# Attention of an fp32 kernel: three products of rounded halves over 128 rows, or whole fp32 over two groups of 64 rows

## The chip, the cores and the metric

One core of a Trainium2 chip runs the whole program in one launch. The metric is the device time of that core in microseconds (us), median of three executions.

## The reference

Attention with rotary embedding, then a mixer of four matrix products. Shapes: 4 batches, 8 heads, 576 positions, head size 64, all float32; the mixer has a hidden size of 256 over positions and of 1536 over channels.

```python
q_rot, k_rot = rotate(q), rotate(k)
scores = (1 / sqrt(64)) * q_rot @ k_rot^T
attn = exp(scores - max(scores));  attn = attn / (sum(attn) + 1e-9)
x = attn @ v                                   # to (4, 576, 512)
u = x + (relu(x^T @ w_tok1) @ w_tok2)^T
out = u + relu(u @ w_ch1) @ w_ch2
```

## The kernel before

The program has two stages, written out by hand with semaphores: attention (function `attention`) and the mixer (function `mixer`, which the change leaves as it is except for the point at which the last sums of attention are taken). Attention runs over 16 pairs `p` of heads, A and B. The 576 queries of each head are 4.5 tiles of 128, so a pair has nine tiles `i`: 0 to 3 are A's, 5 to 8 are B's, and tile 4 holds the last 64 queries of both. Each engine has its own list of steps for a pair, and the order in those lists is the schedule; nothing else moves work.

The steps of a pair are these.

- GpSimd (POOL) rotates q and k (`rotate`, L354 to L362), splits v into halves (`split_v`), and divides the result by the sums (`normalise`).
- TensorE (PE) turns q and k (`transposes`, L585, five matmuls of 128 rows and 128 columns each). ScalarE (ACT) copies what was turned, rounded to fp32r (`t_part_hi`), and VectorE (DVE) takes the rest (`t_part_lo`). Five DMAs per head then lay out `key` (rounded half of k over its rest, 128 rows) and `q_hi`, `q_cross`.
- PE makes the scores of a tile (`score`, L624): four fp32r matmuls of 288 columns, six for tile 4. DVE takes the maximum (`maximum`, L997), ACT the exponent with its sum (`exponent`, L847).
- PE turns the probabilities of the tile (`turn`, L634, four 128 by 128 transposes in fp32; `turn_tails`, L644, for the last 64 keys of two or three tiles at once). ACT copies them rounded (`turned_hi`, L854, and `tails_hi`), DVE takes the rest (`turned_lo`, L1005, and `tails_lo`).
- PE multiplies with v (`values`, L657): v with its rounded half and its rest side by side is the stationary operand, the turned probabilities stream past in four parts of 256 or 320 columns, nine fp32r matmuls each. ACT copies the result (`copy_o`), PE turns it back (`transpose_o`, L383), DVE adds the two halves (`sum_o`).

The score tiles use two PSUM slots of two banks (`slot`); everything else uses the four banks of `rest`, so that several turned tiles can be on their way at once, and `values` of a pair runs during the scores of the next pair. The sums of the last pair are taken inside the mixer (`last_o`, `last_sums`).

A float32 that is rounded to fp32r keeps its upper half; the two halves are multiplied as three products (upper by upper, upper by rest, rest by upper).

```python
passes = ((q_hi[a][:, cols], key[a]), (q_cross[a][:, cols], key[a]))
for n, (queries, keys) in enumerate(passes):
    for f in range(2):
        mm = pe.matmul(s[:, f, 0:HALF], queries, keys[:, f * HALF:(f + 1) * HALF], ...)
```

Of the kernel before, what the change touches and what calls it, by code (L numbers as in the profile page):

```python
# [17 lines left out]
P = 128  # L18
# [3 lines left out]
G = 4  # L22
# [39 lines left out]
def build(nc, q, k, v, w_tok1, w_tok2, w_ch1, w_ch2, rope, x_scratch, out):  # L62
    with ExitStack() as whole:
# [14 lines left out]
        with ExitStack() as placed:  # L78
            sb(placed, "w_ch1_first", [P, CT // 2, CH])
            prob_a = sb(placed, "prob_a", [P, G + 1, S])  # L80
# [61 lines left out]
Attention = namedtuple("Attention", "sync gpsimd tensor scalar vector last_o last_sums last_store buffers_left values_left slot_left")  # L142
# [85 lines left out]
def attention(nc, ctx, whole, sb, slot, rest, ident, stage_or_x, raw_qk, rope_sb, rope_half, prob_a, token, wt1, wt2, w1, x_stored,  # L228
# [7 lines left out]

# [8 lines left out]
    GROUPS = ((0, 2), (2, 5), (5, 7), (7, 9))  # L245
    PARTS = {"A0": (0, 2 * P), "A1": (2 * P, S), "B0": (S, S + HALF + TAIL // 2), "B1": (TILES * P - 2 * P, TILES * P)}
    PV_BANK = {"A0": 0, "A1": 0, "B0": 0, "B1": 2}
    O_BANKS, K_BANKS, Q_BANKS = 1, 2, 2
    EARLY = 2
    EARLY_COLS = (slice(0, EARLY * P), slice(EARLY * P, MAIN))  # L250
    LATE_COLS = slice(EARLY * P, W)

# [3 lines left out]
    rot = {"k": sb(ctx, "rot_k", [P, NG, 2, D])}  # L256
    ot = sb(ctx, "ot", [P, TILES * P])
    O_TILES = {"A": (0, G), "B": (G, TILES)}
    o_sum = {h: sb(ctx, f"o_sum_{h}", [P, O_TILES[h][1] - O_TILES[h][0], D]) for h in "AB"}

    WIDE = {"q": W, "k": S}
    t_hi = {n: [sb(ctx, f"t_hi_{n}{i}", [P, WIDE[n]], F32R) for i in range(2)] for n in "qk"}
    t_lo = {n: [sb(ctx, f"t_lo_{n}{i}", [P, WIDE[n]], F32R) for i in range(2)] for n in "qk"}
    key = [sb(ctx, f"key{a}", [P, S], F32R) for a in range(2)]
    q_cross = [sb(ctx, f"q_cross{a}", [P, MAIN], F32R) for a in range(2)]
    q_hi = [sb(ctx, f"q_hi{a}", [P, MAIN], F32R) for a in range(2)]
# [3 lines left out]
    total = [sb(ctx, f"total{a}", [P, TILES]) for a in range(2)]  # L270
    guarded = [sb(ctx, f"guarded{a}", [P, TILES]) for a in range(2)]
    inverse = [sb(ctx, f"inverse{a}", [P, TILES]) for a in range(2)]
    zeros = sb(ctx, "zeros", [P, NG, D])
    eps = sb(ctx, "eps", [P, TILES])

    rot["q"] = sb(ctx, "rot_q", [P, NG, 2, D])
    raw["v"] = sb(ctx, "raw_v", [P, 2, NG, D])
    prob_b = sb(ctx, "prob_b", [P, G, S])
    prob = [prob_a[:, i, :] for i in range(G + 1)] + [prob_b[:, i, :] for i in range(G)]
    v_sb = [sb(ctx, f"v{a}", [P, NG, P], F32R) for a in range(2)]  # L280
    pt_lo = sb(ctx, "pt_lo", [P, G, TILES * P], F32R)
    pt_hi = sb(ctx, "pt_hi", [P, NG, TILES * P], F32R)
# [4 lines left out]

    tables = sem("rope_tables")
    products = sem("products")
    rotated = sem("rotated")  # L290
    v_hi_done, v_split = sem("v_hi_done"), sem("v_split")
    consts, zero_halves = sem("consts"), sem("zero_halves")
    t_ready, t_hi_done, t_lo_done = ({n: sem(f"{what}_{n}") for n in "kq"} for what in ("t_ready", "t_hi_done", "t_lo_done"))
    tiles_in = [sem(f"tiles_in{a}") for a in range(2)]
    k1_in = sem("k1_in")
    first_turned, first_hi, first_lo = sem("first_turned"), sem("first_hi"), sem("first_lo")

    scores, maxed, exped = sem("scores"), sem("maxed"), sem("exped")
    turned, hi_done, lo_done = sem("turned"), sem("turned_hi_done"), sem("turned_lo_done")
    tails_turned, tails_hi_done, tails_lo_done = sem("tails_turned"), sem("tails_hi_done"), sem("tails_lo_done")  # L300
    pv_ready, ot_done = ({f: sem(f"{what}_{f}") for f in PARTS} for what in ("pv_ready", "ot_done"))
    o_ready, o_summed = ({h: sem(f"{what}_{h}") for h in "AB"} for what in ("o_ready", "o_summed"))
    x_done = sem("x_done")
    guard_done, inv_done = sem("guard_done"), sem("inv_done")
# [4 lines left out]
    ASSEMBLED = 5 * 16  # L309
    STORED = 3 * 16  # L310
    src = {n: a.rearrange("b (g h) s d -> (b g) h s d", h=2) for n, a in (("q", q), ("k", k), ("v", v))}

# [4 lines left out]
    def columns(bank, n):  # L317

        return rest[:].rearrange("p a n -> p (a n)")[:, bank * BANK:bank * BANK + n]

    def first_q(n0, n1):

        if n1 <= EARLY * P:
            return columns(3, n1)[:, n0:n1]
        return columns(2, n1 - EARLY * P)[:, n0 - EARLY * P:n1 - EARLY * P]

    k1_early = prob_b[:].rearrange("p a n -> p (a n)")[:, 0:W].rearrange("p (h t d) -> p h t d", h=2, t=NG)
# [8 lines left out]
    def rotate(eng, n, p):  # L336
# [20 lines left out]
        if p > 0:  # L357
            eng.wait_ge(t_ready[n], p)
        r = rot[n][:].rearrange("p t h d -> p h t d")
        eng.tensor_tensor(r[:, :, :, 0:half], by_cos[:, :, :, 0:half], by_sin[:, :, :, half:D],  # L360
                           ALU.subtract).then_inc(rotated, 1)
        eng.tensor_tensor(r[:, :, :, half:D], by_sin[:, :, :, 0:half], by_cos[:, :, :, half:D],  # L362
                           ALU.add).then_inc(rotated, 1)
# [11 lines left out]

# [3 lines left out]

    def turn_o(pe, h, bank):  # L380

        for n, t in enumerate(range(*O_TILES[h])):
            mm = pe.transpose(columns(bank, W)[:, n * P:(n + 1) * P], ot[:, t * P:(t + 1) * P], ident[:])  # L383
        mm.then_inc(o_ready[h], 1)

    def o_halves(h, bank):

        n = O_TILES[h][1] - O_TILES[h][0]
        return columns(bank, n * P).rearrange("p (t i d) -> p t d i", t=n, i=2)
# [17 lines left out]
    def sync(sp):  # L407
# [14 lines left out]
        def halves(a):  # L422
            top, low = slice(0, D), slice(D, P)
            return (top, low) if a == 0 else (low, top)

        def assemble_q(a, p):

            if no(p):
                return
            i = p % 2  # L430
            mine, other = halves(a)
            sp.wait_ge(t_hi_done["q"], p + 1)
            sp.dma_start(f32(q_hi[a][mine, :]), f32(t_hi["q"][i][mine, 0:MAIN])).then_inc(tiles_in[a], 16)
            sp.dma_start(f32(q_cross[a][other, :]), f32(t_hi["q"][i][mine, 0:MAIN])).then_inc(tiles_in[a], 16)
            sp.wait_ge(t_lo_done["q"], p + 1)
            sp.dma_start(f32(q_cross[a][mine, :]), f32(t_lo["q"][i][mine, 0:MAIN])).then_inc(tiles_in[a], 16)

        def assemble_k(a, p):

            if no(p):  # L440
                return
            i = p % 2
            mine, other = halves(a)
            sp.wait_ge(t_hi_done["k"], p + 1)
            sp.dma_start(f32(key[a][mine, :]), f32(t_hi["k"][i][mine, :])).then_inc(tiles_in[a], 16)
            sp.wait_ge(t_lo_done["k"], p + 1)
            sp.dma_start(f32(key[a][other, :]), f32(t_lo["k"][i][mine, :])).then_inc(tiles_in[a], 16)
# [18 lines left out]
        assemble_k(1, 0)  # L466
        assemble_q(1, 0)
        load("v", 0)
        load_next("k", 2)
        load_next("q", 2)  # L470

        for p in range(N):
            if p > 0:
                sp.wait_ge(v_split, 2 * p)
                load("v", p)
            store(p - 2)
            sp.wait_ge(scores, p * TILES + G)
            assemble_k(0, p + 1)
            assemble_q(0, p + 1)
            load_next("k", p + 3)  # L480
            if p > 0:
                load_next("q", p + 3)
            sp.wait_ge(scores, (p + 1) * TILES)
            assemble_k(1, p + 1)
            assemble_q(1, p + 1)
            if p == 0:
                load_next("q", p + 3)
# [14 lines left out]
        store(N - 2)  # L502

    def gpsimd(pool):
        pool.memset(ident[:], 0.0).then_inc(consts, 1)
        pool.memset(zeros[:], 0.0).then_inc(consts, 1)
        pool.memset(eps[:], 1e-9).then_inc(consts, 1)
        pool.wait_ge(consts, 3)
# [3 lines left out]
        def split_v(p, h):  # L512

            if no(p):
                return
            a = "AB".index(h)
            pool.wait_ge(raw_in["v"], (p + 1) * RAW["v"])
            if p > 0:
                pool.wait_ge(pv_ready[h + "0"], p)
                pool.wait_ge(pv_ready[h + "1"], p)  # L520
            pool.tensor_tensor(v_sb[a][:, :, 0:D], raw["v"][:, a], zeros[:], ALU.add).then_inc(v_hi_done, 1)
            pool.wait_ge(v_hi_done, 2 * p + a + 1)
            pool.tensor_tensor(v_sb[a][:, :, D:P], raw["v"][:, a], f32(v_sb[a][:, :, 0:D]),
                               ALU.subtract).then_inc(v_split, 1)

        def guard(p):

            if no(p):
                return
            pool.wait_ge(exped, (p + 1) * TILES)  # L530
            if p >= 2:
                pool.wait_ge(inv_done, p - 1)
            pool.tensor_tensor(guarded[p % 2][:], total[p % 2][:], eps[:], ALU.add).then_inc(guard_done, 1)

        def normalise(p, h):

            if no(p):
                return
            a = "AB".index(h)
            pool.wait_ge(inv_done, p + 1)  # L540
            pool.wait_ge(o_summed[h], p + 1)
            if h == "B" and p > 0:
                pool.wait_ge(x_stored, p * STORED)
            t0, t1 = O_TILES[h]
            pool.tensor_tensor(x_pair[:, 1 - a:NG, a, :], o_sum[h][:],
# [1464 lines left out]
```

## Time and profile before

| | |
|---|---|
| median of 3 executions (range) | 639.42 us (639.29 to 639.71) |
| the profiled execution: its own time, its span | 639.26 us, 637.4 us |
| PE busy, share of the span, instructions | 621.5 us, 98%, 4724 |
| PE weight loads busy | 604.5 us, 95%, 4724 |
| DVE busy | 509.9 us, 80% |
| ACT busy | 465.2 us, 73% |
| POOL busy | 341.4 us, 54% |
| DMA: bytes, mean rate | 62.32 MB, 98 GB/s |

Busy time counts the stretch in which an instruction is recorded on its engine. Matmuls overlap, and each is recorded with its latency, so what a matmul costs is read from the distance between two starts, not from its own duration. The same holds to a smaller degree for the other engines. The profiled execution lies 1.9 us outside its span and 0.2 us under the median.

### The profile page before, as it was taken

To read this page: it belongs to the slowest core of one execution; us is meant where nothing else is said; L and a number is where in the kernel's file an instruction comes from. 1 tells how busy PE (TensorE), PEld (TensorE's weight loads), DVE (VectorE), ACT (ScalarE), POOL (GpSimd) and SP (SyncE) were. 2 spreads that over 40 slices of the span, in tenths; PEclk is the share of its full clock that TensorE was granted. 3 is DMA by queue.
4 is the path that set the end of the run, shared out by engine and by line. 5 is a ranking of instruction groups with operands and counts; after the bars stand their busy time and mean duration, and the time that the engine had idled before them with its cause. 6 is when DMAs were issued, how large, how long until landed. Compare 5 with 4: busy or idle time off the path is not lost.

```text
span 637.4 us, 13799 instructions
## 1 busy us (share of the span) xinstructions
PE 621.5 (98%) x4724; PEld 604.5 (95%) x4724; DVE 509.9 (80%) x881; ACT 465.2 (73%) x1018; POOL 341.4 (54%) x316
## 2 busy tenths in 40 slices
PE   4899999999999999999999999999999999999997
PEld 3799999999999999999999999999999999999997
DVE  7899999999999999977385985569935499553895
ACT  5888999988888999976383655776556765567753
POOL 4999999998888887551900002860017800068200
PEclk9999999999999999999999999999999999999999
DMA  4667766676668765406002331000320003100002
GB/s 130 177 152 205 199 161 169 170 188 172 168 180 212 206 172 127 110 20 217 20 1 64 136 99 60 1 2 2 84 75 0 0 0 82 48 27 2 0 3 74
DMA packets 59594, 62.32 MB, mean 98 GB/s; under 512 B 16592, under 2 KB 43856, under 8 KB 59536
## 3 DMA queue, kind: packets, MB, share of 16 engines
q1 hardware_dynamic: 59232, 61.50, 35.4%
q8 instruction: 34, 0.56, 0.3%
q14 instruction: 24, 0.20, 0.1%
q10 hardware_dynamic: 304, 0.07, 0.0%
HBM read 30.77 MB, written 9.44 MB: 63 GB/s over the span
## 4 chain that ended last, share of the span: by engine, by line
PE 95%; DVE 1%; POOL 1%; ACT 1%; issue 0%
PE slot L624 12%; PE rest L657 12%; PE rest L634 9%; PE slot L1359 8%; PE slot L1361 8%; PE slot L1360 8%; PE rest L1359 6%; PE rest L1361 6%; PE rest L1360 6%; PE rest L383 3%; PE rest L585 3%; PE rest L644 2%; PE slot L1391 2%; PE rest L1391 2%; PE rest L224 1%; PE rest L221 1%
## 5 line engine op out<-in xcount | busy, mean ns | idle before, releaser
L1350 POOL TENSOR_TENSOR w_ch_part<-w_ch_sums,w_ch_part 128x512 fp32r<-128x512 f32 x21 | 31.0, 1476 | 173.3 <-ACT w_ch_part L1603 173.3
L997 DVE TENSOR_REDUCE neg_max<-slot 128x1 f32<-128x576 f32 x142 | 106.7, 752 | 6.3 <-PE slot L624 2.0
L1667 ACT ACTIVATE pieces<-h 128x288 fp32r<-128x288 f32 x168 | 73.8, 444 | 49.8 <-PE slot L1361 24.5
L1005 DVE TENSOR_TENSOR pt_lo<-rest,pt_hi 128x512 fp32r<-128x512 f32 x144 | 96.0, 677 | 1.8 <-ACT pt_hi L854 1.3
L657 PE MATMUL rest<-pt_hi,v 128*128 128x256 f32 (+1 forms) x320 | 89.3, 303 | 0.0
L854 ACT ACTIVATE pt_hi<-rest 128x512 fp32r<-128x512 f32 x144 | 84.1, 596 | 5.1 <-PE rest L634 4.2
L1758 DVE TENSOR_TENSOR pieces<-h,pieces 128x288 fp32r<-128x288 f32 x168 | 74.4, 453 | 9.3 <-ACT pieces L1667 8.8
L657 PE MATMUL rest<-pt_lo,v 128*128 128x256 f32 (+1 forms) x256 | 69.7, 295 | 0.0
L847 ACT ACTIVATE prob_a<-slot,neg_max 128x576 f32<-128x576 f32 x78 | 57.9, 743 | 9.8 <-DVE neg_max L997 9.6
L624 PE MATMUL slot<-key,q_hi 128*128 128x288 f32 x252 | 63.5, 333 | 1.5 <-ACT prob_a L847 0.5
L657 PEld LDWEIGHTS rest<-pt_hi,v 128*128 128x128 f32 x320 | 60.3, 188 | 0.2
L624 PE MATMUL slot<-key,q_cross 128*128 128x288 f32 x252 | 54.0, 296 | 0.0
L657 PEld LDWEIGHTS rest<-pt_lo,v 128*128 128x128 f32 x256 | 48.3, 189 | 0.0
L847 ACT ACTIVATE prob_b<-slot,neg_max 128x576 f32<-128x576 f32 x64 | 47.4, 741 | 0.3 <-DVE neg_max L997 0.2
L354 POOL TENSOR_TENSOR by_cos<-raw_qk,rope_sb 128x640 f32<-128x640 f32 x29 | 45.3, 1561 | 2.0
L634 PE MATMUL rest<-ident,prob_a 128*128 128x128 f32 x320 | 45.5, 273 | 0.6 <-DVE t_lo_q L986 0.5
L1825 DVE TENSOR_TENSOR h<-h 128x288 f32<-128x288 f32 x96 | 42.6, 452 | 3.9 <-ACT h L1566 3.8
L355 POOL TENSOR_TENSOR by_sin<-raw_qk,rope_sb 128x640 f32<-128x640 f32 x29 | 45.5, 1569 | 0.0
L624 PEld LDWEIGHTS slot<-key,q_hi 128*128 128x128 f32 x252 | 38.6, 193 | 3.1 <-ACT prob_a L847 1.0
L624 PEld LDWEIGHTS slot<-key,q_cross 128*128 128x128 f32 x252 | 40.5, 190 | 0.0
L634 PEld LDWEIGHTS rest<-ident,prob_a 128*128 128x128 f32 x320 | 37.9, 141 | 1.4 <-DVE t_lo_q L986 0.7
L634 PE MATMUL rest<-ident,prob_b 128*128 128x128 f32 x256 | 38.3, 273 | 0.4 <-DVE pt_lo L1005 0.2
(268 smaller groups left out, 2109.3 us busy)
## 6 DMA issues: line engine op xcount, KB each, us to landing
key<-t_hi_k SPq DMA_DIRECT2D x31, 144.0 KB, 2.3
key<-t_lo_k SPq DMA_DIRECT2D x31, 144.0 KB, 2.4
raw_qk<-in_q_dram SPq DMA_DIRECT2D x16, 256.0 KB, 2.6
raw_v<-in_v_dram SPq DMA_DIRECT2D x16, 256.0 KB, 3.1
x_scratch<-x_pair SPq DMA_DIRECT2D x16, 256.0 KB, 2.2
stage_or_x<-x_scratch SPq DMA_DIRECT2D x16, 256.0 KB, 4.1
q_hi<-t_hi_q SPq DMA_DIRECT2D x31, 128.0 KB, 2.4
q_cross<-t_hi_q SPq DMA_DIRECT2D x31, 128.0 KB, 2.4
```

The source lines that it names most:

```text
L624: mm = pe.matmul(s[:, f, 0:HALF], queries, keys[:, f * HALF:(f + 1) * HALF], start=(n == 0), stop=(n == len(passes) - 1))
L634: mm = pe.transpose(rest[:, bank, j * P:(j + 1) * P], prob[i][:, j * P:(j + 1) * P], ident[:])
L657: mm = pe.matmul(rest[:, PV_BANK[f], 0:n1 - n0], v_sb[a][:, j, :], pt[:, j, n0:n1], start=(j == 0 and pt is pt_hi), stop=(j == NG - 1))
L847: act.activation(prob[i].rearrange("p (f n) -> p f n", f=2), s[:, :, 0:HALF], ACT.Exp, bias=neg_max[p % 2][:, i:i + 1], accum_out=total[p ...
L854: act.activation(pt_hi[:, 0:G, i * P:(i + 1) * P], rest[:, bank, :].rearrange("p (j n) -> p j n", j=G), ACT.Copy).then_inc(hi_done, 1)
L997: dve.tensor_reduce(neg_max[p % 2][:, i:i + 1], slot[g if 2 <= g < 4 else g % 2][:, :, 0:HALF], AX.XY, ALU.max, negate=True).then_inc(maxe ...
L1005: dve.tensor_tensor(pt_lo[:, :, cols], rest[:, bank, :].rearrange("p (j n) -> p j n", j=G), f32(pt_hi[:, 0:G, cols]), ALU.subtract).then_i ...
L1359: pe.matmul(ps, lhs[0], rhs[0], start=first, stop=False, skip_group_check=True)
L1360: pe.matmul(ps, lhs[0], rhs[1], start=False, stop=False, skip_group_check=True)
L1361: return pe.matmul(ps, lhs[1], rhs[0], start=False, stop=last, skip_group_check=True)
L1667: act.activation(pieces[:, ring(m), 0, :], source[WEIGHTS[n]][:, ft, :], ACT.Copy).then_inc(piece_hi, 1)
L1758: dve.tensor_tensor(pieces[:, ring(m), 1, :], source[WEIGHTS[n]][:, ft, :], f32(pieces[:, ring(m), 0, :]), ALU.subtract).then_inc(piece_lo, 1)
```

## The change

Attention is written anew, with the same pairs and tiles. Every matmul of it, transposes too, now uses 64 rows of the array, and neighbours use the upper and the lower 64 rows in turn and write to different PSUM banks. No operand is split into halves.

- Scores: two fp32 matmuls of 288 columns per tile (four for tile 4). For half of the keys q and k are used where the transposition left them, for the other half a copy in the other 64 partitions, made by one DMA for q and one for k per head (`move`).
- Turned tiles: ten transposes of 64 rows by 128 columns with a 64 by 64 identity (`half_turn`), all into `rest[:, 0:2]`. One copy of 128 x 640 takes a tile out, on ACT for tiles 0, 2, 4, 6, 8 and on DVE for 1, 3, 5, 7 (`copy_turned`); the next tile is turned once that copy is done. q and k are turned into the two score slots, in line with the tiles.
- Values: the turned probabilities are now the stationary operand, 64 rows of 128 columns, and v streams past with a column of ones (65 columns), so that the sum of the exponents comes out beside the result and nothing is turned back. A pair has 90 such matmuls, into `rest[:, 2:4]`, one bank for each group of rows; DVE adds the two banks (`sum_o`), after head A's tiles and after head B's.
- The copies of v, q and k are single, the halving by ACT and DVE and the reads of the accumulated sums are gone, `last_o` and `last_sums` too.

```diff
-                    mm = pe.matmul(s[:, f, 0:HALF], queries, keys[:, f * HALF:(f + 1) * HALF],
-                                   start=(n == 0), stop=(n == len(passes) - 1))
+                for r, (x, w) in enumerate((own(0), other(1)) if a == 0 else (other(0), own(1))):
+                    mm = pe.matmul(s[:, r, 0:HALF], x[:, cols], w, start=True, stop=True, skip_group_check=True)
...
+        def half_turn(to, x, r):
+            rows = (top, low)[r]
+            return pe.matmul(to, x, ident[rows, rows], start=True, stop=True, is_transpose=True, skip_group_check=True)
...
-        def turn(p, i, bank):
+        def turn(p, i):
...
+                copied(pe, g - 1)
+            pe.wait_ge(exped, g + 1)
...
-            for j in range(G):
-                mm = pe.transpose(rest[:, bank, j * P:(j + 1) * P], prob[i][:, j * P:(j + 1) * P], ident[:])
+            for j in range(NG):
+                for r, rows in enumerate((top, low)):
+                    at = j * P if j < G or (i in UPPER and (i, r) != (G, 0)) else S - P
+                    x = wide[i][rows, at:at + P]
+                    mm = half_turn(rest[:, r, j * D:(j + 1) * D], x, r)
...
-                for pt in ((pt_hi, pt_lo) if j < G else (pt_hi,)):
-                    mm = pe.matmul(rest[:, PV_BANK[f], 0:n1 - n0], v_sb[a][:, j, :], pt[:, j, n0:n1],
-                                   start=(j == 0 and pt is pt_hi), stop=(j == NG - 1))
+            elif i == 0:
+                pe.wait_ge(o_summed["B"], p)
...
+                return pe.matmul(rest[:, 2 + r, at:at + V], x[rows, j, :], w[rows, j, :], start=begins, stop=ends, skip_group_check=True)
...
+        for p in range(N):
+            score(p, 0)
+            turn(p - 1, 7)
+            values(p - 1, 6)
             score(p, 1)
+            turn(p - 1, 8)
+            values(p - 1, 7)
             score(p, 2)
+            turn(p, 0)
+            values(p - 1, 8)
+            transposes("k", p + 1)
+            turn(p, 1)
+            values(p, 0)
             score(p, 3)
+            turn(p, 2)
             score(p, 4)
+            values(p, 1)
+            turn(p, 3)
             score(p, 5)
+            values(p, 2)
+            transposes("q", p + 1)
+            turn(p, 4)
+            values(p, 3)
             score(p, 6)
+            score(p, 7)
+            turn(p, 5)
+            values(p, 4)
             score(p, 8)
+            turn(p, 6)
+            values(p, 5)
...
-            dve.tensor_tensor(pt_lo[:, :, cols], rest[:, bank, :].rearrange("p (j n) -> p j n", j=G),
-                              f32(pt_hi[:, 0:G, cols]), ALU.subtract).then_inc(lo_done, 1)
+            dve.tensor_copy(pt_of(p, i)[:].rearrange("p j (r n) -> p j r n", r=2),
+                            banks_by_rows(rest[:, 0:2])).then_inc(by_dve_done, 1)
```

On PE, here is one stretch of a pair before, from the third score tile to the first part of the values (rows of `rest` from `pt_hi`, `pt_lo` are the products with v).

```order
L624 MATMUL slot<-key,q_hi 128x288 [waits exped]
L624 MATMUL slot<-key,q_hi 128x288
L624 MATMUL slot<-key,q_cross 128x288 x2
L657 MATMUL rest<-pt_hi,v 128x256 [waits turned_lo_done,tails_lo_done,v_split]
L657 MATMUL rest<-pt_lo,v 128x256
L657 MATMUL rest<-pt_hi,v 128x256
```

The same place now: from the third score tile of a pair to its first values.

```order
L611 MATMUL slot<-turned_k,turned_q 128x288 [waits exped]
L611 MATMUL slot<-moved_k,moved_q 128x288
L550 MATMUL rest<-ident,prob_a 128x64 [waits exped,turned_copied_by_act]
L550 MATMUL rest<-ident,prob_a 128x64 x9
L653 MATMUL rest<-v,pt 128x65 [waits turned_copied_by_act]
L653 MATMUL rest<-v,pt 128x65 x9
L550 MATMUL slot<-ident,rot_k 128x64 [waits rotated,exped]
L550 MATMUL slot<-ident,rot_k 128x64 x9
L550 MATMUL rest<-ident,prob_a 128x64 [waits exped,turned_copied_by_act]
L550 MATMUL rest<-ident,prob_a 128x64 x9
L653 MATMUL rest<-v,pt 128x65 [waits v_copied,o_summed_B,turned_copied_by_act]
L653 MATMUL rest<-v,pt 128x65 x7
```

Each turned tile now waits for the copy of the one before it, and the values of tile 0 wait for the sum of the pair before.

On DVE before, the steps of a pair after the second and third maximum (L997), down to the sixth.

```order
L997 TENSOR_REDUCE neg_max<-slot 128x1 [waits scores] x2
L1013 TENSOR_TENSOR pt_hi<-rest,pt_hi 64x384 [waits tails_hi_done]
L989 TENSOR_TENSOR t_lo_k<-rest,t_hi_k 128x576 [waits t_hi_done_k]
L1005 TENSOR_TENSOR pt_lo<-rest,pt_hi 128x4x128 [waits turned_hi_done]
L997 TENSOR_REDUCE neg_max<-slot 128x1 [waits scores]
L1005 TENSOR_TENSOR pt_lo<-rest,pt_hi 128x4x128 [waits turned_hi_done]
L986 SCALAR_TENSOR_TENSOR t_lo_q<-rest,t_hi_q 128x640 [waits t_hi_done_q]
L997 TENSOR_REDUCE neg_max<-slot 128x1 [waits scores]
```

And now, from the maxima of tiles 1 and 2 to that of tile 5.

```order
L844 TENSOR_REDUCE neg_max<-slot 128x1 [waits scores] x2
L864 TENSOR_REDUCE y_B<-rest 128x325 [waits x_done,o_added]
L836 COPY turned_k<-slot 128x640 [waits tiles_in1,tiles_in0,t_ready_k]
L854 COPY pt<-rest 128x640 [waits o_added,turned]
L872 TENSOR_TENSOR guarded<-y_B,eps 128x5 [waits o_summed_B]
L844 TENSOR_REDUCE neg_max<-slot 128x1 [waits scores]
L881 RECIPROCAL inverse<-guarded 128x5 [waits x_done,guard_done]
L844 TENSOR_REDUCE neg_max<-slot 128x1 [waits scores]
L854 COPY pt<-rest 128x640 [waits o_added,turned]
L844 TENSOR_REDUCE neg_max<-slot 128x1 [waits scores]
```

The sum of head B, the copy of k and the copy of turned tile 1 now stand in one row on DVE, between the maxima of tiles 2 and 3.

## Rows read from the trace of the kernel before

**Rows 1.** The page's first part: busy time, share of the span, instructions

```profile
PE 621.5 (98%) x4724; PEld 604.5 (95%) x4724; DVE 509.9 (80%) x881; ACT 465.2 (73%) x1018; POOL 341.4 (54%) x316
```

**Rows 2.** Windows: one pair, attention, mixer; busy us (x instructions), clock, DMA share, GB/s

```profile
150.43:167.59 17.16, 17.16 (x140) 16.65 (x139) 16.58 (x27) 15.27 (x38) 14.54 (x16) 1.00 0.70 181
12.00:297.00 285.00, 281.95 (x2215) 270.20 (x2214) 267.99 (x434) 255.61 (x611) 234.57 (x238) 1.00 0.63 166
297.00:637.40 340.40, 336.14 (x2501) 331.68 (x2499) 233.13 (x427) 204.44 (x401) 103.55 (x69) 1.00 0.13 40
```

**Rows 3.** Chain that ended last, over one pair: shares, then pieces (start us, us, what)

```profile
by line: PE slot L624 31.2%; PE rest L657 27.7%; PE rest L634 22.9%; PE rest L383 6.7%; PE rest L585 6.4%; PE rest L644 5.7%; issue 0.0%
...
150.43 0.55 PE rest L585 x5
150.97 0.44 PE rest L634 x4
...
153.43 0.52 PE slot L624 x4
...
160.97 1.07 PE rest L657 x9
```

**Rows 4.** Groups of weight loads by shape: count, busy us, mean ns of one

```profile
L624 PEld LDWEIGHTS slot<-key,q_hi 128*128 128x128 f32 x252 | 38.6, 193 | 3.1 <-ACT prob_a L847 1.0 <-DMA q_cross<-t_lo_q 0.9 <-issue 0.7
L634 PEld LDWEIGHTS rest<-ident,prob_b 128*128 128x128 f32 x256 | 29.8, 141 | 1.4 <-DVE pt_lo L1005 0.5 <-ACT ot L874 0.4
L644 PEld LDWEIGHTS rest<-ident,prob_b 128*64 128x64 f32 x64 | 6.9, 110 | 0.8
```

**Rows 5.** Timeline: two loads behind each other after a wait, transposes, then fp32r

```profile
287.83 0.20 PEld L634 LDWEIGHTS rest<-ident,prob_b 128*128 128x128 f32 x2 [0.41 <-ACT ot L874]
...
17.60 0.30 PEld L624 LDWEIGHTS slot<-key,q_hi 128*128 128x128 f32 x2 [0.42 <-ACT prob_a L847]
```

**Rows 6.** Timeline: two matmuls of a score tile, and the maximum that waits for them

```profile
17.98 0.43 PE L624 MATMUL slot<-key,q_cross 128*128 128x288 f32 x2
...
18.44 0.76 DVE L997 TENSOR_REDUCE neg_max<-slot 128x1 f32<-128x576 f32 x1 [0.78 <-PE slot L624]
```

**Rows 7.** Timeline of DVE: steps without a wait between them

```profile
153.12 0.75 DVE L997 TENSOR_REDUCE neg_max<-slot 128x1 f32<-128x576 f32 x1
153.78 0.68 DVE L1005 TENSOR_TENSOR pt_lo<-rest,pt_hi 128x512 fp32r<-128x512 f32 x1
154.38 0.81 DVE L986 SCALAR_TENSOR_TENSOR t_lo_q<-rest,t_hi_q 128x640 fp32r<-128x640 f32 x1
155.11 0.75 DVE L997 TENSOR_REDUCE neg_max<-slot 128x1 f32<-128x576 f32 x1
```

**Rows 8.** Timeline of ACT: steps without a wait between them

```profile
153.47 0.71 ACT L834 ACTIVATE t_hi_q<-rest 128x640 fp32r<-128x640 f32 x1
154.07 0.74 ACT L847 ACTIVATE prob_a<-slot,neg_max 128x576 f32<-128x576 f32 x1
154.69 0.20 ACT L847 ACTIVATION_READ_ACCUMULATOR prob_a<-slot,neg_max 128x1 f32 x1
```

**Rows 9.** Groups of DVE and POOL by shape: count, busy us, mean ns of one

```profile
L1022 DVE TENSOR_REDUCE o_sum_B<-rest 128x320 f32<-128x640 f32 x15 | 12.4, 825 | 1.6 <-PE rest L383 1.5
L355 POOL TENSOR_TENSOR by_sin<-raw_qk,rope_sb 128x640 f32<-128x640 f32 x29 | 45.5, 1569 | 0.0
L360 POOL TENSOR_TENSOR rot_q<-by_cos,by_sin 128x320 f32<-128x320 f32 x15 | 13.2, 883 | 1.2
L521 POOL TENSOR_TENSOR v<-raw_v,zeros 128x320 fp32r<-128x320 f32 x32 | 28.0, 875 | 15.6 <-PE rest L657 15.6
L545 POOL TENSOR_TENSOR x_pair<-o_sum_B,inverse 128x320 f32<-128x320 f32 x16 | 11.6, 725 | 17.4 <-DVE o_sum_B L1128 13.5 <-issue 4.0
```

**Rows 10.** Timeline of PE: the nine transposes of the last result, in the mixer

```profile
299.54 1.15 PE L383 MATMUL rest<-ident,ot 128*128 128x128 f32 x9
```

More of the change, by code:

```diff
@@ L277, in attention @@
+    rot["q"][0] = sb(ctx, "rot_q0", [P, NG, 2, D])
     raw["v"] = sb(ctx, "raw_v", [P, 2, NG, D])
[L278 to L282, printed above, removed]
+    prob_b = sb(ctx, "prob_b", [P, G * S + 2 * TAIL])
+    starts = {0: 0, 1: S, 2: 2 * S + TAIL, 3: 3 * S + TAIL, G: 4 * S + 2 * TAIL, 5: 0, 6: S, 7: 2 * S + TAIL, 8: 3 * S + TAIL}
@@ L420, in load_next, with move @@
             load(n, p)
[L422 to L426, printed above, removed]
+        def move(n, a, p):
             if no(p):
                 return
[L430 to L447, printed above, removed]
+            here, there = ((top, low), (low, top))[a]
+            sp.wait_ge(t_done[n], p + 1)
+            sp.dma_start(moved_x[n][there, :], turned_x[n][p % 2][here, MOVED_COLS[n][a]]).then_inc(tiles_in[a], 16)
         def store(p):
@@ L612, in score, with own, other @@
+            queries, keys = (turned_x[n][p % 2] for n in "qk")
+            def own(r):
+                rows = (top, low)[r]
+                return queries[rows], keys[rows, r * HALF:(r + 1) * HALF]
+            def other(r):
+                rows = (top, low)[r]
+                return moved_x["q"][rows], moved_x["k"][rows, :]
             if i == G:
-                cols, b = slice(MAIN, W), p % 2
-                passes = ((t_hi["q"][b][:, cols], t_hi["k"][b]), (t_hi["q"][b][:, cols], t_lo["k"][b]),
-                          (t_lo["q"][b][:, cols], t_hi["k"][b]))
+                cols = slice(MAIN, W)
+                for n, halves in enumerate(((own(0), other(1)), (other(0), own(1)))):
+                    for r, (x, w) in enumerate(halves):
+                        mm = pe.matmul(s[:, r, 0:HALF], x[:, cols], w, start=(n == 0), stop=(n == 1), skip_group_check=True)
@@ L635, in turn, with values @@
             mm.then_inc(turned, 1)
[L637 removed]
+        def values(p, i):
             if no(p):
                 return
[L641 to L659 removed]
@@ L728, in tensor @@
+            mm.then_inc(o_added, 1)
+        pe.wait_ge(consts, 2)
+        transposes("k", 0)
+        transposes("q", 0)
+        for p in range(N):
+            score(p, 0)
+            turn(p - 1, 7)
+            values(p - 1, 6)
             score(p, 1)
-            after_sum(p - 2, "B")
-            transpose_o(p - 2, "A")
+            turn(p - 1, 8)
+            values(p - 1, 7)
             score(p, 2)
-            after_lo(p - 1, 4)
-            values(p - 1, "A0", 2, 1)
-            after_sum(p - 2, "A")
@@ L1063, in vector @@
[L1063 to L1078 removed]
+        copy_k(0)
+        dve.wait_ge(t_done["k"], 1)
@@ L1517, in body @@
                 u_unit(b, c, begins)
-                if begins and c == 0:
-                    first.last_o(pe)
             if begins:
```

710 lines of the change are left out of this document (250 added, 460 removed).

## Prediction

> **What bounds the kernel now.** I read the busy shares first, then the two stages apart, then the chain of waits in one pair, because the change touches attention alone. PE is busy for 98% of the span [rows 1], and attention takes 285 us of it, the mixer 340 us [rows 2]. Inside attention a pair repeats every 17.16 us, from one turning of k (150.43) to the next (167.59), and PE is busy in all of it, while DVE has 16.58 us and ACT 15.27 us of work there; the granted clock is 1.00, that is 2.4 GHz, throughout [rows 2]. The chain of that pair is PE from end to end with 0.0% of issue [rows 3]. So what counts is the distance between matmul starts. By the shares a pair spends 31.2% on scores, 27.7% on values, and 41.7% on turning (L634, L585, L644, L383) [rows 3]: 5.3, 4.7 and 7.1 us. DVE has only 0.6 us of slack, so a PE that got faster alone would gain little; the change takes work off both.
>
> **Prices of TensorE.** The trace gives these. A transpose of 128 columns starts every 0.109 us (0.44 for four, 0.55 for five), four score matmuls of 288 columns take 0.52 us, 0.13 each, and nine value matmuls of 256 columns take 1.07 us, 0.12 each [rows 3]. In fp32r that is about 0.45 ns per column; in an fp32 transpose 0.85 ns.
>
> Not shown before: (a) an fp32 matmul that is no transpose, (b) two matmuls in different row groups, (c) a weight load for one. For (a): the kernel now multiplies two halves by two halves in three products; whole fp32 has four, so a matmul streams four times the fp32r columns, at least 4 x 0.41 x 288 = 0.47 us for 288 columns (0.41 from 0.13 us less some 12 ns that do not grow with columns, by the difference of 0.133 and 0.119 us for 288 and 256), and at most 4 x 0.13 = 0.53. I take 0.50. For 65 columns it is 4 x 0.41 x 65 = 0.108. For (b): from side by side (two for the price of one) to one after the other; I take side by side, since loads and matmuls of unlike operands overlap all through the trace. For (c) the two nearest rows differ. Two loads for fp32 transposes take 0.20 us together, one 0.141, so they start 57 ns apart; two for fp32r take 0.30, one 0.193, so 108 ns apart [rows 4, 5]. The load for 64 columns is 0.110 against 0.141 [rows 4], so columns set it. A whole fp32 product would need its stationary halves one after the other, two loads per matmul. I take 57 ns, by the fp32 row, since the operand type is that one's; 108 is the other end.
>
> The Trainium skill, "TensorEngine Tiling (Array Packing)", Key Properties, states that different tiles of the array can load weights and multiply in parallel. No row here shows it; it speaks for the forecast's end of (b).
>
> **The change on PE, per pair.** Turning: nine tiles, q and k, ten half transposes each; a pair of them streams 64 columns, 0.055, and is held by its load, 0.057: 11 x 5 x 0.057 = 3.1 us, for 7.1. Scores: 8 tiles of one pair of matmuls and tile 4 of two: 10 x 0.50 = 5.0, for 5.3. Values: 90 matmuls, 45 pairs, two loads of 0.057 against 0.108 of streaming: 45 x 0.114 = 5.1, for 4.7. Sum 13.2 us for 17.16.
>
> **Who is late next.** The other engines fall too. DVE: a maximum occupies it 0.66 to 0.68, a 640-column step from PSUM 0.73 [rows 7]; 9 maxima, 4 tile copies, the copy of k, the two sums (0.76 and 0.62, by 825 ns for 640 elements less the overlap of 0.07) [rows 9] and some 0.5 of small steps give 11.6 us. ACT: exponent 0.62 to 0.64, 640-column copy 0.60 [rows 8]: 9 x 0.64 + 5 copies and q at 0.60 to 0.75 = 9.5. The nine accumulator reads of 0.20 each are gone. POOL: 2 x (2 x 1.57 + 2 x 0.88) + 2 x 0.875 at most + 1.34 = 12.9 [rows 9], under any period here; it is cover only down to that. The moves are four DMAs instead of ten, with over 2 us to spare before the tile that needs them; SP passes nothing that PE waits for.
>
> But the turned tile has one place, and the value sums too, so PE must wait. A reader of PSUM starts 0.19 us after the last matmul's turn ends (17.98 + 2 x 0.133 = 18.25, the maximum at 18.44) [rows 6]; I add 0.10 from the end of a copy to PE's next matmul. I walked one pair through the four lists of steps with these numbers. The waits that come out:
> - The turn of tile 8 waits for DVE's copy of tile 7, which stands behind maximum 0 (0.68 to 1.36, copy to 2.16, PE again at 2.26 against 1.88): 0.38 us.
> - The values of tile 0 wait for the sum of head B: 0.19 + 0.83 + 0.10 after the last values, of which 0.71 is covered by turning k and tile 1: 0.41 us.
> - The turn of tile 2 waits for the copy of tile 1, on DVE behind that sum (to 5.34) and the copy of k (to 6.07), done at 6.87: 0.51 us.
> - Score 6 waits for exponent 5, since maximum 5 stands behind the copy of tile 3: 0.46 us.
> - The turn of tile 5 waits for tile 4's double copy on ACT (0.21), score 7 for the copy of q (0.12), and four small ones 0.3: 0.6 us.
>
> Together 2.4 us, so a pair takes 13.2 + 2.4 = 15.6 us, 1.5 us less than before. Sixteen pairs give 24 us. The nine transposes of the last result inside the mixer (1.15 us recorded, 1.0 of it their turn) go as well [rows 10]. Start and end of attention I leave equal: first scores need the same two rotations and a copy for the other rows. Sum, against the profiled execution of 639.3 us: 639.3 - 24 - 1 = 614. The profiled execution is 0.2 us under the median, which I leave out.
>
> **Rivals.**
> 1. *The loads cost what fp32r's cost.* If each half of the stationary operand takes 108 ns [rows 5], the values are 45 x 2 x 0.108 = 9.7 us instead of 5.1, while scores hide their loads behind 0.25 us of streaming and transposes keep 57. PE then has 17.9 to 18.4 us, the waits shrink to about 0.6 since PE itself is late, and a pair takes 19.0: 16 x 1.8 - 1 = +28, **667 us**. It decides once a load costs over 80 ns. For it: 193 ns in the very engine and stage; against it: those are fp32r operands. The Trainium skill, "TensorE: Matmul & The Clock Gate", LDWEIGHTS (loading the stationary operand), gives columns divided by 1.2, about 107 ns for 128 columns whatever the rows; the fp32r loads agree, the 57 ns of the transposes do not.
> 2. *Loads of the two row groups go one after another.* Each load at 57 ns: turning 110 x 0.057 = 6.3, values 180 x 0.057 = 10.3, scores 5.0: 21.5 us, +4.3 a pair, **707 us**.
> 3. *The row groups don't run side by side at all*: scores 10.0 too, 26.5 us a pair, +9.3, **787 us**. Nothing in the trace excludes 2 or 3, so both keep a chance; against 3 stands that weight loads and matmuls already run beside each other all through the trace (PE 98% and loads 95% busy) [rows 1].
> 4. *One place for the turned tile binds.* If copies take 0.2 us more than I said or start later, nine of them in a row add up to 1.5 us and the gain is gone: **640 us**. For it: the four copies on DVE stand behind maxima. Against it: 2.4 us of waits are already in the sum.
> 5. The change could compute its scores no faster (0.53 instead of 0.50) and each small matmul cost 5 ns more than streaming: +0.3 and +0.5 us on PE, half of it in the waits: 622. That is within the forecast.
>
> **How the numbers follow.** Forecast 0.60, with its own range of 602 (waits of 1.6 us instead of 2.4) to 632; rival 1 0.22; rival 2 0.09; rival 3 0.05; rival 4 0.04. Predicted 614. The range 602 to 672 takes in the forecast, rivals 4 and 1, and leaves out 2 and 3 and a little below. Faster by over 0.2% (which is what a measurement of this kernel can tell from no change) 0.60, within it 0.03, slower 0.37.
>
> **What would show it.** The distance between pairs in attention falls from 17.16 to about 15.6 us; PE busy falls to near 85% there, and its idle time names the copies of DVE at the turns of tiles 8 and 2, the sum of head B and exponent 5. Ten half transposes take 0.29 us, ten value matmuls 0.57, a score tile 0.50. Loads 57 ns apart and in pairs at nearly the same start say (b) and (c) are right. Ten value matmuls at 1.1 us mean rival 1 (if ten half transposes stay at 0.29) or rival 2 (if these take 0.57). The mixer should keep its 340 us; if it doesn't, part of my sum is wrong.

## The result, and the profile after

The changed kernel takes 675.5 us (median of 4 executions, 673.3 to 676.0), the kernel before in the same series 639.6: a ratio of 1.056, interval 1.053 to 1.058. The forecast of 614 had the wrong sign, and the time lies 3.5 us above the upper end of the range. Rival 1 (the loads cost what fp32r's cost), with its 667, is the one that happened. Most executions of a kernel agree within 0.3%; where one lies over 1.5% above the kernel's fastest, as in experiments 1 and 6, both are given and only the faster counts.

The page's first part and the windows of the changed kernel answer to [rows 1, 2]; in the windows come one pair, attention and the mixer:

```profile
PE 650.6 (97%) x7796; PEld 622.2 (92%) x7796; DVE 436.7 (65%) x764; ACT 383.5 (57%) x677; POOL 295.3 (44%) x276
...
161.89:181.09 19.20, 18.85 (x337) 17.55 (x334) 12.15 (x21) 10.29 (x16) 11.95 (x14) 1.00 0.41 112
...
12.00:334.00 322.00, 314.73 (x5293) 291.00 (x5293) 198.09 (x324) 176.03 (x275) 189.22 (x193) 1.00 0.40 108
334.00:674.00 340.00, 334.30 (x2483) 329.99 (x2483) 231.04 (x425) 203.88 (x399) 102.25 (x67) 0.99 0.11 37
```

What the change was to take off DVE, ACT and POOL, it took: a pair has 12.15, 10.29 and 11.95 us of work there, for 16.58, 15.27 and 14.54. None of it shows in the time, because PE is still busy nearly all the time (18.85 of 19.20 us), and it now needs 19.20 us for a pair instead of 17.16. Sixteen times 2.04 are 32.6 of the 36.8 us by which the span grew. The mixer kept its 340.

The chain of waits over one pair, answering to [rows 3] (start us, us, what; shares by line first):

```profile
by line: PE rest L653 53.0%; PE slot L611 22.2%; PE rest L550 14.4%; PE slot L607 5.3%; PE slot L550 3.2%; issue 1.8%
...
161.89 0.31 PE slot L550 x10
162.21 0.32 PE rest L550 x10
162.52 1.12 PE rest L653 x20
163.64 1.02 PE slot L611 x8
...
164.97 2.01 PE rest L653 x36
166.98 0.54 PE slot L611 x4
...
175.00 0.35 issue
```

L653 are the value matmuls, L611 and L607 the scores, L550 every half transpose. The profile records a whole fp32 matmul as two loads and two matmuls, so "x20" are ten matmuls, five in each row group, and "x4" is the pair of matmuls of one score tile. By the shares a pair spends 10.2 us on values, 5.3 on scores, 3.4 on turning and 0.35 in one idle stretch. The stretch stands ahead of the values of tile 0, where the profile names no releaser; the timeline shows DVE's sum of head B, for which these values wait, end 0.10 us before they start:

```profile
174.42 0.84 DVE L864 TENSOR_REDUCE y_B<-rest 128x325 f32<-128x650 f32 x1 [0.67 <-PE rest L653]
175.36 1.11 PE L653 MATMUL rest<-v,pt 64*128 64x65 f32 x16 [0.35 <-issue]
```

Do the two row groups run side by side? The timeline of PE shows two lines for each step of a score tile, with starts 0.01 us apart (start us, duration, then the instruction):

```profile
160.34 0.46 PE L611 MATMUL slot<-moved_k,moved_q 64*128 64x288 f32 x1
160.35 0.46 PE L611 MATMUL slot<-turned_k,turned_q 64*128 64x288 f32 x1
```

They do, and the loads with them (160.28 and 160.29 us for this step). The groups of weight loads, against [rows 4], are of 64 rows and 128 columns:

```profile
L653 PEld LDWEIGHTS rest<-v,pt 64*128 64x128 f32 x2304 | 145.9, 190 | 9.9 <-issue 7.3
...
L550 PEld LDWEIGHTS rest<-ident,prob_a 64*128 64x128 f32 x800 | 35.9, 144 | 6.3 <-DVE pt L854 3.1 <-issue 0.5 <-ACT pt L770 0.4
```

The load of a value matmul is recorded with 190 ns, that of a transpose of the same shape with 144. These are the two kinds of [rows 4], 193 and 141, and the value matmuls' loads are of the slow kind although nothing is rounded.

### The profile page after: what moved, and what is told of

It reads as the page before. It is cut to its first block, busy times and chain, and to the rows that moved or that the text cites. A ratio compares the mean times of both kernels' runs of the same rounds, so it can differ in the third digit from the quotient of the medians.

```text
span 674.2 us, 19213 instructions
## 1 busy us (share of the span) xinstructions
PE 650.6 (97%) x7796; PEld 622.2 (92%) x7796; DVE 436.7 (65%) x764; ACT 383.5 (57%) x677; POOL 295.3 (44%) x276
## 4 chain that ended last, share of the span: by engine, by line
PE 96%; issue 1%; DVE 1%; ACT 1%; DVEq 0%
PE rest L653 24%; PE slot L611 10%; PE slot L1157 8%; PE slot L1159 8%; PE slot L1158 8%; PE rest L550 7%; PE rest L1157 6%; PE rest L1159 6%; PE rest L1158 6%; PE slot L607 3%; PE slot L1189 2%; PE rest L1189 2%; PE slot L550 1%; PE rest L224 1%; PE rest L221 1%
## 5 line engine op out<-in xcount | busy, mean ns | idle before, releaser
L653 PE MATMUL rest<-v,pt 64*128 64x65 f32 x2304 | 151.8, 273 | 5.6 <-issue 5.6
L653 PEld LDWEIGHTS rest<-v,pt 64*128 64x128 f32 x2304 | 145.9, 190 | 9.9 <-issue 7.3
L770 ACT ACTIVATE pt<-rest 128x640 f32<-128x640 f32 x64 | 45.0, 703 | 85.8 <-PE rest L550 85.8
L611 PE MATMUL slot<-turned_k,turned_q 64*128 64x288 f32 x256 | 88.2, 436 | 2.3 <-ACT moved_q L785 1.6
L611 PE MATMUL slot<-moved_k,moved_q 64*128 64x288 f32 x256 | 88.2, 436 | 0.0
L854 DVE COPY pt<-rest 128x640 f32<-128x640 f32 x64 | 52.3, 817 | 11.7 <-PE rest L550 11.7
L611 PEld LDWEIGHTS slot<-turned_k,turned_q 64*128 64x128 f32 x256 | 40.6, 192 | 3.6 <-issue 1.8
L550 PEld LDWEIGHTS rest<-ident,prob_a 64*128 64x128 f32 x800 | 35.9, 144 | 6.3 <-DVE pt L854 3.1
L611 PEld LDWEIGHTS slot<-moved_k,moved_q 64*128 64x128 f32 x256 | 40.7, 192 | 1.1
L550 PE MATMUL rest<-ident,prob_a 64*128 64x64 f32 x800 | 40.1, 226 | 0.3 <-ACT pt L770 0.3
L550 PEld LDWEIGHTS rest<-ident,prob_b 64*128 64x128 f32 x640 | 31.5, 139 | 8.3 <-issue 0.4
```

The source lines that it names most:

```text
L550: return pe.matmul(to, x, ident[rows, rows], start=True, stop=True, is_transpose=True, skip_group_check=True)
L611: mm = pe.matmul(s[:, r, 0:HALF], x[:, cols], w, start=True, stop=True, skip_group_check=True)
L653: return pe.matmul(rest[:, 2 + r, at:at + V], x[rows, j, :], w[rows, j, :], start=begins, stop=ends, skip_group_check=True)
L770: ins = act.activation(pt_of(p, i)[:].rearrange("p j (r n) -> p j r n", r=2), halves, ACT.Copy)
L854: dve.tensor_copy(pt_of(p, i)[:].rearrange("p j (r n) -> p j r n", r=2), banks_by_rows(rest[:, 0:2])).then_inc(by_dve_done, 1)
```

## The experiments

The theories were these. **L**: each of the two loads of a value matmul takes about 110 ns in its row group and sets the pace. **S**: the matmuls stream slower than 65 columns by my price. **F**: each pass has a fixed cost whatever its columns. Two more came up on the way: what a change of the array's division costs, and why the start was slow.

### 1. Half the streamed columns

```diff
-  return pe.matmul(rest[:, 2 + r, at:at + V], x[rows, j, :], w[rows, j, :], ...)
+  return pe.matmul(rest[:, 2 + r, at + 32:at + V], x[rows, j, :], w[rows, j, 32:V], ...)
```

> The changed kernel, but the value matmuls stream 33 columns (the last 32 of v and the ones) instead of 65, so half of the result is left out. Theory L (each half of the fp32 stationary operand costs a load of some 110 ns per group of rows, and that sets the pace): nothing changes, 673 to 677 us, twenty value matmuls still 1.12 us. Theory S (the streaming of small fp32 matmuls is slower than 108 ns for 65 columns): the pace falls by up to half, twenty in 0.6 to 0.9 us, a pair 2 to 4 us shorter, 610 to 645 us. Theory F (a fixed cost for each matmul of a group of rows, whatever its columns): nothing changes, as L.

Measured: 681.6 and 696.7 us. Most pairs keep the pitch, 19.17 to 19.20 us, and so do the value groups:

```profile
129.38 1.98 PE rest L653 x36
...
137.69 1.09 PE rest L653 x20
```

With 33 columns instead of 65 they take 1.98 and 1.09 us, for 2.01 and 1.12. So S falls: streaming was hidden. The kernel is nevertheless slower, since in four stretches of about 3 us (from 42, 120, 198 and 315 us) matmuls run at half pace. The granted clock falls to 0.50 there, the 1.2 GHz level, while PE is busy. The eight score halves that take 1.02 us elsewhere take twice that:

```profile
121.53 2.01 PE slot L607 x8
...
121.50:123.50 2.00, 2.00 (x14) 1.71 (x12) 0.38 (x2) 1.34 (x2) 1.53 (x2) 0.52 0.03 3
```

A pair with such a stretch takes 20.8 us. Four times 1.6 us are 6.4, about the 6.1 by which 681.6 lies above the changed kernel. Why the clock falls is not shown.

### 2. One load and one pass

Turned probabilities and v are rounded to fp32r, and their rests are left out, so the products are less exact than in either kernel; v has 66 columns instead of 65.

```diff
-    V = D + 1
+    V = D + 2
-    v_sb = [sb(ctx, f"v{a}", [P, NG, V]) for a in range(2)]
+    v_sb = [sb(ctx, f"v{a}", [P, NG, V], F32R) for a in range(2)]
-    pt = [sb(ctx, f"pt{i}", [P, NG, P]) for i in range(TURNED)]
+    pt = [sb(ctx, f"pt{i}", [P, NG, P], F32R) for i in range(TURNED)]
...
```

> [...] Theory L: 90 loads instead of 180 at the same 112 ns, values 5.0 us a pair instead of 10.05, PE 13.8 us and about 2 us of waits (my walk with these numbers gives 15.8 a pair): 16 x 3.4 less, 621 us (614 to 630). Theory F with the cost once per matmul instruction as written (not per pass): nothing, 675. Theory that the load of a whole fp32 operand is dearer than that of fp32r: values fall below 5 us, 615 or less.

Measured: 623.9 us, ratio to before 0.975 (0.972 to 0.978). Ten value matmuls now take 0.55 us, five per row group, 110 ns each for one load of 128 columns; 66 columns in one pass would stream in some 30 ns, an estimate by the 0.45 ns of an fp32r column. The pair takes 15.93 us. The chain of waits, over one pair:

```profile
78.99 0.64 issue
79.64 0.83 DVE pt L854
...
82.36 0.55 PE rest L653 x10
...
82.94 0.06 DVE y_B L864
...
83.70 0.82 DVE turned_k L836
...
88.65 0.76 DVE neg_max L844
...
89.43 0.75 ACT prob_b L755
```

With the loads halved, the waits that the forecast had named are back: DVE's copies of turned tiles (L854), the sum of head B (L864), the copy of k (L836), and a maximum with its exponent. This run comes near the forecast's world: values cost PE about 5 us, though with one load and one pass for each product. In three of its later pairs another wait shows that I had ruled out:

```profile
155.20 3.73 DMA moved_q<-turned_q
```

Where this DMA is on the chain the pair takes 16.4 to 16.5 us instead of 15.9. I had given it "over 2 us to spare".

### 3. 64 stationary columns in most value matmuls

```diff
+  n0 = P if begins else D
-  return pe.matmul(rest[:, 2 + r, at:at + V], x[rows, j, :], w[rows, j, :], ...)
+  return pe.matmul(rest[0:n0, 2 + r, at:at + V], x[rows, j, 0:n0], w[rows, j, :], ...)
```

In 72 of the 90 matmuls of a pair the upper 64 queries of a tile are left out.

> The changed kernel, but 72 of the 90 value matmuls of a pair load 64 stationary columns instead of 128 (the first of each sum keeps 128), so most of the result for 64 of 128 queries is left out. Theory L: those loads cost some 56 ns and the streaming of 65 columns, 54 ns a pass, sets the pace with them: values 9 x 0.224 + 36 x 0.115 = 6.2 us instead of 10.05; by the walk a pair takes 16.4 us instead of 19.2, 630 us (620 to 640). Theory F: nothing, 675. Theory S: nothing, 675.

Measured: 711.6 us, ratio 1.112 (1.108 to 1.116), pitch 21.5. The groups did not all go one way:

```profile
159.13 1.31 PE rest L654 x36
160.43 0.69 PE slot L611 x4
...
161.42 0.72 PE rest L654 x16
...
163.14 1.74 PE rest L654 x20
```

The group of 36 fell from 2.01 to 1.31 and that of 16 from 0.90 to 0.72, but that of 20, where widths of 64 and 128 alternate, rose from 1.12 to 1.74, and each score tile behind a value group costs 0.69 for 0.54. The run missed its expectation because I had taken a change of width as free. It suggested a price for one of 0.2 to 0.3 us, which the next runs were to measure.

### 4. 64 columns in all value matmuls, from the second pair on

```diff
+  n0 = P if p == 0 else D
-  return pe.matmul(rest[:, 2 + r, at:at + V], x[rows, j, :], w[rows, j, :], ...)
+  return pe.matmul(rest[0:n0, 2 + r, at:at + V], x[rows, j, 0:n0], w[rows, j, :], ...)
```

> The changed kernel, but all value matmuls of every pair after the first load 64 stationary columns and not 128 (the values of the upper 64 queries of each tile are left out there), so that the width no longer changes inside a group of value matmuls, only between such a group and the turns and scores around it. If a load sets the pace of the value matmuls by its columns, they start 56 ns apart in each row group, a group of 20 takes 0.56 us plus one change (0.27), so nine groups take 5.0 + 2.4 us for 10.05, and the pair 16.5 to 17.5 us: 635 to 650. If a matmul costs 112 ns for another reason (a fixed cost of each pass), the groups keep 10.05 us and the changes come on top: about 700 to 715.

Measured: 645.6 us, ratio 1.009 (1.007 to 1.011), pitch 17.23. The chain of waits:

```profile
149.72 0.73 PE rest L654 x20
150.45 1.17 PE slot L611 x8
...
151.93 1.20 PE rest L654 x36
153.13 0.69 PE slot L611 x4
...
154.12 0.61 PE rest L654 x16
```

The three sizes of group have 18, 10 and 8 loads per row group. 1.20, 0.73 and 0.61 us lie on one line: 58 to 59 ns for each load, plus 0.15 us. In the changed kernel the same groups give 112 ns per load (2.01 / 18, 1.12 / 10). So the time of these matmuls goes with the columns of the stationary operand: 112 ns for 128, 58 for 64. Streaming is close behind there (54 ns for 65 columns, by the 0.24 us between recorded matmuls of 288) and could be the floor, so 58 is an upper bound for the load. The recorded loads agree: those of 64 columns have a mean of 134 ns, for 190 before, 56 ns less:

```profile
L654 PEld LDWEIGHTS rest<-v,pt 64*64 64x64 f32 x2160 | 72.9, 134 | 21.7 <-issue 16.4 <-ACT pt L771 0.3
```

F falls, L stands. The 0.15 us come once on going in, and once more in the step behind (0.69 for 0.54, 1.17 for 1.02).

With 0.15 a change the odd group of the run before works out: it has five changes (0.75), two matmuls alone at each width (2 x 2 x 0.058 + 2 x 2 x 0.112 = 0.68) and three pairs (6 x 0.058 = 0.35), together 1.78 against 1.74.

### 5. 128 rows and 64 rows in turn

The changed kernel, with five full transposes for q and k instead of ten halves from the second pair on; the copies of q and k on ACT and DVE read them in one piece.

```diff
+  if p > 0:
+      for t in range(NG):
+          mm = pe.transpose(to.rearrange("p a n -> p (a n)")[:, t * P:(t + 1) * P], rot[n][p % 2][:, t].rearrange("p h d -> p (h d)"), ident[:])
```

> The changed kernel, but q and k of every pair after the first are turned with transposes of all 128 rows (five each, as before the change) in place of ten half transposes. Their own price is 0.109 us each, so PE gets 2 x (0.55 - 0.31) = 0.48 us more per pair. Theory that changing between 64 and 128 rows costs nothing: pitch 19.7 us, time about 675.5 + 15 x 0.48 = 683. Theory that each change of the array's division costs what the run with 64 stationary columns showed at its changes of width (0.2 to 0.3 us): four changes per pair, +1.0 more, pitch 20.7, time about 698.

Measured: 682.4 us, ratio 1.067 (1.065 to 1.070), pitch 19.74.

```profile
163.15 0.70 PE slot L575 x5
163.84 0.46 PE rest L550 x10
```

The time is what the theory without a price gave, 683, and that theory is wrong: the rows show the price. Five full transposes take 0.70 for 0.55 in [rows 3], and the ten halves behind them 0.46 for 0.31: 0.15 us on each side. Twice a pair that is 2 x (0.39 + 0.15) = 1.08 us more, of which the idle stretch of 0.35 and a value group (0.94 for 1.11) gave back half: PE reaches the values of tile 0 at 177.32, after the sum of head B, which ran from 176.21 for 0.84 us. A total that fits is no proof of the terms.

The same from the other side: the kernel before, with the nine transposes of the result made as 18 halves, read back from two banks.

```diff
-  mm = pe.transpose(columns(bank, W)[:, n * P:(n + 1) * P], ot[:, t * P:(t + 1) * P], ident[:])
+  for r, rows in enumerate((slice(0, D), slice(D, P))):
+      mm = pe.matmul(rest[:, bank + r, n * D:(n + 1) * D], ot[rows, t * P:(t + 1) * P], ident[rows, rows], ..., is_transpose=True)
...
```

> The kernel before, with one part of the change alone: the nine transposes per pair that turn the result back are made as 18 half transposes of 64 rows, two side by side, into two banks. By the half transposes' own price (0.062 us a pair of them against 0.109) PE has 0.42 us less per pair and the time falls by 15 x 0.42 = 6 to about 633.5. If a change between 64 and 128 rows costs 0.2 to 0.3 us, four of them per pair give +1.0 - 0.4 = +0.6 us a pair: about 649.

Measured: 640.3 us, ratio 1.0007 (0.9997 to 1.0016), between the two expectations.

```profile
164.14 0.46 PE rest L384 x10
164.60 0.59 PE rest L636 x4
165.19 0.53 PE slot L626 x4
165.72 0.39 PE rest L384 x8
166.11 0.72 PE slot L626 x4
```

The ten halves take 0.46, that is 0.31 + 0.15, for 0.55 before; the four full transposes behind them 0.59 for 0.44. The saving is paid back by the second change, and nothing is left. Half transposes pay only where the work around them uses 64 rows too, as in the changed kernel.

### 6. Four matmuls of one row group, then four of the other

```diff
                 for j in range(G):
                     add(0, i, pt_of(p, i), v_sb[a], j, begins=(j == 0), ends=(j == G - 1))
+                for j in range(G):
                     add(1, i, pt_of(p, i), v_sb[a], j, begins=(j == 0))
...
```

> The changed kernel with the same value matmuls, but the four of the upper rows of a tile stand together and then the four of the lower rows, instead of in turn (not for tile 4). If two groups of rows work at once only while neighbours in the list differ (matmuls start in order), the eight tiles cost up to twice: 72 loads each way at 112 ns, values up to 18 us a pair, 760 to 800 us. If the queue lets the lower group run ahead over four matmuls of the upper one: 675 to 690 us.

Measured: 887.1 us in the profiled execution, 732.0 in the other. The 732.0 lies between the two expectations; at full pace a pair takes 22.2 us for 19.2. So the row groups still overlap, but only in part. Up to about 364 us the profiled execution ran at half pace, 40.9 us a pair, and one group of value matmuls reads like this there and later on:

```profile
73.25 2.37 PE rest L653 x17
...
369.60 1.28 PE rest L653 x17
```

The column of the granted clock reads 1.00 all the same in the slow stretch (windows from 60 to 80 and from 300 to 340 us); its first reading below that stands between 376 and 378 us, and it is no proof of full speed, as experiment 8 shows. What held the pace down for so long is open.

### 7. PE kept busy at the start

38 transposes of the identity, which nobody reads, in the time in which PE waits for q and k.

```diff
+  def warm(n):
+      for _ in range(n):
+          pe.transpose(slot[1][:, 1, 384:512], ident[:], ident[:])
   pe.wait_ge(consts, 2)
+  warm(24)
   transposes("k", 0)
+  warm(7)
   transposes("q", 0)
+  warm(7)
```

> The changed kernel with 38 more full transposes of the identity, whose results nobody reads, on PE in its idle time at the start: 24 ahead of the first turning of k, 7 ahead of that of q, 7 ahead of the first score. If the half pace of matmuls up to 24.5 us comes from PE having been mostly idle until then, full pace begins some 8 to 10 us earlier and the time falls by about 4 to 5 us, to 671. If the half pace belongs to these matmuls or to the start of the program, the time stays at 675.5 or rises by up to 1.

Measured: 671.9 us, ratio to before 1.050 (1.048 to 1.052), 3.6 us less than the changed kernel. The timeline of the changed kernel, score halves with 0.48 us between starts as late as 23 us:

```profile
22.38 0.68 PE L607 MATMUL slot<-turned_k,turned_q 64*128 64x288 f32 x1
...
22.86 0.68 PE L607 MATMUL slot<-turned_k,turned_q 64*128 64x288 f32 x1
```

and of this run, where full pace begins at about 14.0 and the same score halves are 0.24 apart:

```profile
19.89 0.40 PE L607 MATMUL slot<-turned_k,turned_q 64*128 64x288 f32 x1
...
20.13 0.40 PE L607 MATMUL slot<-turned_k,turned_q 64*128 64x288 f32 x1
```

PE was busy for 1.60 us of the first 12 in the changed kernel, for 3.41 in the kernel before, whose score matmuls reach their full pace at 14.4, and for 8.41 in this run.

### 8. Rounded, and busy at the start

> The two edits that helped, together: turned probabilities and values rounded to fp32r (one load and one pass per value matmul), and the 38 unread transposes at the start. If they act apart, the time is 623.9 less the 3.6 us that the transposes gave the changed kernel: 620.3. If the rounded kernel's first pair is bound by waits and not by PE's pace, less comes back: 621 to 624.

Measured: 623.2 us (621.1 to 625.5), ratio to before 0.974 (0.971 to 0.976). That cannot be told from the 623.9 without the extra transposes, and the trace says why: the transposes didn't bring full pace here, though PE was busy for 7.73 us of the first 12. Score halves are still 0.48 us apart at 22 us (starts at 21.61 and 22.10), as in experiment 2. From 14 to 22 us both runs do the same work in the same time, yet the column of the granted clock differs (this run, then experiment 2):

```profile
14.00:22.00 8.00, 7.00 (x64) 0.50 0.41 108
...
14.00:22.00 8.00, 7.00 (x64) 1.00 0.44 114
```

So neither expectation was tested as it was meant: the time lies within the second, "621 to 624", but by a slow start and not by waits. The five executions go with their mean granted clock, from 621.1 us at 0.996 to 625.5 at 0.987. The rounded kernel is the fastest of the study either way.

## Why the prediction was wrong, step by step

| step, per pair | forecast | measured | where |
|---|---|---|---|
| turning, 110 half transposes | 3.1 us | 3.4 | shares of the chain |
| scores, 10 pairs of matmuls | 5.0 | 5.3 | shares of the chain |
| values, 90 matmuls | 5.1 | 10.2 | shares of the chain |
| waits of PE | 2.4 | 0.35 | the issue piece |
| pair | 15.6 | 19.2 | distance between turnings of k |

**The step that failed is price (c)**, the load for a whole fp32 matmul: I took 57 ns, by the row of the fp32 transposes, "since the operand type is that one's". It is 112 ns, the fp32r end (108). Two loads per matmul make 45 x 2 x 0.112 = 10.1 us of values instead of 5.1. The type did not decide. The fast loads are those of the transposes, and every matmul that multiplies has slow ones, in either type; [rows 4, 5] already held both kinds, but each type stood there with one kind of work only, and I read the difference as one of type. Experiments 1, 2 and 4 show it: streaming half the columns gained nothing, one load instead of two gave 0.55 for 1.12 us, 64 stationary columns gave 58 ns per load at most. The Trainium skill, "TensorE: Matmul & The Clock Gate", LDWEIGHTS section, gives columns divided by 1.2, an estimate of 107 ns for 128 columns and 53 for 64. The 112 agrees with it, the 58 as an upper bound does not contradict it, the transposes' 62 ns per pair of halves do not agree. I had quoted that rule and given it 0.22.

**Price (a)**, four passes per fp32 product, was right in size: a score tile takes 0.54 with 0.48 of it streaming; the forecast was 0.50 and its upper bound 0.53. The 0.41 ns per column does not follow from the difference that the prediction cites (0.014 us for 32 columns is 0.44), but 0.24 us for two passes of 288 columns is 0.42. **Price (b)**, side by side, was right, for matmuls and loads; rivals 2 and 3 fall by the starts 0.01 us apart. Ten half transposes take 0.31 for 0.29.

**The waits** were right as a mechanism. In the changed kernel they shrink, as rival 1 said, since PE is late itself. The one that is left is the second of the forecast's list, the sum of head B before the values of tile 0: 0.35 us for 0.41. (The 0.71 us of cover in that term has no source; the two turnings named there are 0.57.) In experiment 2, where values take about 5 us, PE's waits name the copies of DVE and exponents of head B, and the pair takes 15.93 us against the 15.6 of the forecast. What the walk missed is `moved_q`. Rival 4 (one place for the turned tile) adds a part there and nothing in the changed kernel; its 640 leaves out the 1 us of the mixer that the other sums take off.

**The sum of rival 1** was 19.0 a pair, near the measured 19.2, and 667 in all. Its PE time is 17.8 by its own terms, not 17.9, which changes nothing. The 8.5 us that are missing: 16 x 0.2 = 3.2 for the pair, and 3.6 at the start, where I left start and end of attention equal and PE stayed at half pace longer after more idle time (experiment 7 gives it back, experiment 8 does not, so what decides it is open). About 1 us is in the mixer, which should have gained 1 from the transposes that went. PE waits there for 0.86 us behind DVE's `h_lo` (at 334.44 us), where the kernel before went straight on. At the end of attention, steps of the mixer with 128 rows stand between those with 64 and pay for changes too (0.43 for 0.24 twice, 0.46 for 0.31), 0.5 us. No run separates the last two.

**The range** fell short by 3.5 us: it ended 5 above rival 1, and rival 1 had no width of its own.

## What to carry to other kernels

A matmul of few streamed columns, 65 here, costs what its stationary operand costs to load, not what it streams. Before splitting work into 64-row groups, count loads: whole fp32 needs two for each product, and with 65 streamed columns they cost twice the streaming. Keep the operand that is reused stationary and stream many columns past it, or round so that one load does where the result allows it, and price a load only from a row of the same kind of work (a transpose says nothing about a product). An edit that relieves three engines is worth nothing while the fourth is the bound and gets slower.

## What the runs showed of the hardware

- A change between 128 and 64 rows, or between 128 and 64 stationary columns, costs 0.15 us each way, in four kernels (experiments 3, 4, 5 and its counterpart). The Trainium skill, "TensorEngine Tiling (Array Packing)", Key Properties, says that changing the tiling mode drains TensorE. The 0.15 us fits that, but the runs show only the time and not what it is made of.
- Two row groups of 64 load and multiply side by side in fp32 if their instructions alternate; in blocks of four a pair takes 16% longer (22.2 us for 19.2).
- Matmuls can run at half pace where the column of the granted clock reads 1.00: up to about 25 us in the changed kernel, for over 300 us in experiment 6. The windows of the first of these stretches:

```profile
18.00:24.00 6.00, 6.00 (x52) 5.05 (x52) 2.08 (x3) 1.81 (x3) 5.84 (x7) 1.00 0.39 104
```

  PE is busy in all of it, yet each step takes about twice its later time. The column does say it in the four stretches of experiment 1, at the start of experiment 8, and in experiment 7, where the stretch is short:

```profile
12.00:14.00 2.00, 2.00 (x10) 0.50 0.68 160
```

  0.50 is the 1.2 GHz level. Since experiment 8 reads 0.50 over the very work and times that read 1.00 in experiment 2, a 1.00 in this column can be a missing reading, and the distance between equal matmuls is the safer one.
